# An early tile of the fullest expert between dense part and routed loop, and logits of three row tiles in three column groups

## The reference

```python
def _attn_ref(q, k, v, g_norm):
    kv = np.einsum('bhsd,bhse->bhde', k, v)
    out = np.einsum('bhsd,bhde->bhse', q, kv)
    rms = np.sqrt(np.mean(out * out, axis=-1, keepdims=True) + 1e-06)
    return out / rms * g_norm

def _moe_ref(x, domain_probs, w1, w2):            # every expert, every row
    p = domain_probs / (domain_probs.sum(-1, keepdims=True) + 1e-09)
    for e in range(E):
        out += p[:, e:e + 1] * (np.maximum(x @ w1[e], 0.0) @ w2[e])

def _moe2_ref(x, expert_emb, tau, w1, w2):        # one expert for each row
    logits = xn @ en.T / tau                      # xn, en: rows over their norms
    expert_idx = np.argmax(logits, axis=1)
    gate_w = softmax(logits)[np.arange(N), expert_idx]
    for e in range(E):
        mask = expert_idx == e
        out[mask] = gate_w[mask, None] * (np.maximum(x[mask] @ w1[e], 0.0) @ w2[e])
```

## Time and profile before

| | |
|---|---|
| runs before, median of 3 | 1151.87 us (1150.92 to 1154.58) |
| the profiled execution | 1151.53 us |
| its span | 1149.9 us, 18699 instructions |
| PE busy | 1125.5 us, 98% of the span |
| DVE, POOL, ACT busy | 728.5 (63%), 655.9 (57%), 455.3 us (40%) |
| mean granted clock of PE | 0.994 |
| HBM traffic | 218 GB/s over the span |

### The profile page before, as it was taken

One profiled execution on the slowest core, in us unless ns is written; L12 is line 12 of the kernel. 1 busy time (PEld: TensorE's weight loads), 2 busy tenths in 40 slices (PEclk: granted clock), 3 DMA queues, 4 the chain that ended last, 5 costly groups with the idle time before them and its releaser, 6 DMA issues.

```text
span 1149.9 us, 18699 instructions
## 1 busy us (share of the span) xinstructions
PE 1125.5 (98%) x6206; PEld 992.3 (86%) x6207; DVE 728.5 (63%) x1159; ACT 455.3 (40%) x808; POOL 655.9 (57%) x609
## 2 busy tenths in 40 slices
PE   8999999999999999999999999999999999999996
PEld 8888889999889888998889888998887788888885
DVE  4877888888976788888875878888662222222221
ACT  4773444444434444444434444444222222222220
POOL 1587777799867777899867777777330111111101
PEclk9999999999999999999999999999989999999998
DMA  9955777777512448877612448777369749427960
GB/s 245 268 157 180 267 268 271 278 275 276 199 45 78 142 131 302 289 278 261 216 37 75 137 146 302 279 273 270 144 243 383 273 183 372 153 100 302 374 238 13
DMA packets 102433, 250.87 MB, mean 218 GB/s; under 512 B 8254, under 2 KB 48190, under 8 KB 94171
## 3 DMA queue, kind: packets, MB, share of 16 engines
q1 hardware_dynamic: 97360, 235.18, 59.2%
q0 software_dynamic: 4800, 14.72, 3.7%
q10 hardware_dynamic: 203, 0.05, 0.0%
HBM read 170.99 MB, written 79.98 MB: 218 GB/s over the span
## 4 chain that ended last, share of the span: by engine, by line
PE 82%; DVE 7%; POOL 4%; issue 3%; DMA 2%; ACT 2%; SPq 0%; DVEq 0%; POOLq 0%; ACTq 0%
PE ps L1277 25%; PE ps L1279 25%; PE ps L1278 25%; PE ps L1466 2%; DMA w_raw<-in_moe_w_dram 1%; DVE x_rows L965 1%; POOL w_lo L483 1%; PE ps L1235 1%; PE ps L1432 1%; PE ps L1370 1%; DVE hT_lo L954 1%; PE ps L1205 1%; DVE attn_rows L887 1%; DVE x_ops_lo L978 1%; DVE hT_lo L952 0%
## 5 line engine op out<-in xcount | busy, mean ns | idle before, releaser
L1277 PE MATMUL ps<-x_ops_hi,w_hi 128*128 128x384 f32 x672 | 226.5, 337 | 3.4 <-DVE sum L935 3.2
L1277 PE MATMUL ps<-w_hi,hT_hi 128*128 128x512 f32 x576 | 227.1, 394 | 0.4
L1279 PE MATMUL ps<-x_ops_hi,w_lo 128*128 128x384 f32 x672 | 225.7, 336 | 0.0
L1279 PE MATMUL ps<-w_hi,hT_lo 128*128 128x512 f32 x576 | 225.4, 391 | 0.0
L1278 PE MATMUL ps<-x_ops_lo,w_hi 128*128 128x384 f32 x672 | 225.2, 335 | 0.0
L1278 PE MATMUL ps<-w_lo,hT_hi 128*128 128x512 f32 x576 | 225.0, 391 | 0.0
L965 DVE SCALAR_TENSOR_TENSOR x_rows<-ps,dense_probs,x_rows 128x512 f32<-128x512 f32 x270 | 189.8, 738 | 22.2 <-PE ps L1279 22.2
L608 POOL DMA_INDIRECT out_dram<-y_rows,row_ids x22 | 22.6, 1026 | 237.3 <-DVE y_rows L1168 141.9
L492 POOL TENSOR_TENSOR w_lo<-w_raw,w_hi 128x512 fp32r<-128x512 f32 x96 | 149.5, 1577 | 8.0 <-ACT w_hi L702 8.0
L1158 DVE TENSOR_TENSOR rhT_lo<-ps,rhT_hi 128x512 fp32r<-128x512 f32 x44 | 28.4, 686 | 172.9 <-ACT rhT_hi L826 172.9
L478 POOL TENSOR_TENSOR w_lo<-w_raw,w_hi 128x512 fp32r<-128x512 f32 x48 | 62.2, 1295 | 126.7 <-ACT w_hi L690 126.6
(11 more groups left out here) (198 smaller groups left out, 2006.8 us busy)
## 6 DMA issues: line engine op xcount, KB each, us to landing
w_slots<-split_parts SPq DMA_DIRECT2D x64, 1024.0 KB, 5.6
w_raw<-in_moe_w_dram SPq DMA_DIRECT2D x96, 512.0 KB, 3.5
ahead_raw<-in_moe_w_dram SPq DMA_DIRECT2D x64, 512.0 KB, 6.6
split_parts<-ahead_hi SPq DMA_DIRECT2D x64, 512.0 KB, 4.4
split_parts<-ahead_lo SPq DMA_DIRECT2D x64, 512.0 KB, 5.8
row_tile<-dispatched_rows POOLq DMA_DIRECT2D x20, 257.0 KB, 5.8
kv<-in_k_dram SPq DMA_DIRECT2D x16, 288.0 KB, 7.9
kv<-in_v_dram SPq DMA_DIRECT2D x16, 288.0 KB, 8.2
```

The source lines that it names most:

```text
L1277: mm(out_, ah, bh, start=(first and m == 0), stop=False, skip_group_check=not final or not first)
L1279: last = mm(out_, al, bh, start=False, stop=(final and m == n - 1), skip_group_check=not final or not first)
```

## The change

It does two things.

**An early tile.** At step 41, when twelve of the row tiles are routed and scattered, DVE picks the expert that leads (`choose_star`, 13 small instructions) and shifts that expert's region and tables by one tile. SP loads 128 of its rows; in the tail PE flips them, and ACT and DVE split them. SP loads the w1 of that expert (`load_early(0)`) into the pieces of the odd place ahead of the w1 of place 0, and after the last down product its w2 (`load_early(1)`). PE computes the tile where the fillers were, with pieces of the work between the last ranks; ReLU, copies and splits of it are placed between routing and table steps on ACT and DVE. `tile 0` is now this tile, the loop's tiles start with 1, and two of them are written out ahead of the loop. The w1 of place 1 and both w2 are loaded behind the first row tiles. The last six tiles' scatters count on a semaphore of their own.

**Logits of the first four blocks.** The embeddings, padded with zeros to 32 columns, are the stationary operand, and the flipped tiles move, 128 columns each. The three tiles of a block write to partitions 0, 32 and 64 of one bank. ACT copies the 96 x 128 result and PE transposes it once. The buffer of flipped tiles has three places in place of two. The last six tiles keep the old form.

The diff, cut to its core:

```diff
+            def load_early(m):
+                for c in range(PCS):
+                    n = (2 * m + 1) * PCS + c
+                    sp.dma_start(W[:, n * PIECE:(n + 1) * PIECE].bitcast(F32),
+                                 parts[e_star, :, (m * PCS + c) * PIECE:(m * PCS + c + 1) * PIECE]).then_inc(early_in[m][c // 2], 16)
...
                     fill_rows()
-            sp.wait_ge(up_done, OPS * STEPS)
+            sp.wait_ge(star_ready, 1)
+            e_star = sp.value_load(tab_s[0:1, 0:1], min_val=0, max_val=E2 - 1)
+            r_star = sp.value_load(tab_s[0:1, 1:2], min_val=P, max_val=E2 * CAP)
             for s in range(2):
                 sp.wait_ge(s_out[s], 32 * (NAHEAD // 2))
-            for n in range(2 * PCS):
-                load_first(n)
+            sp.wait_ge(scattered, 16 * T0)
+            sp.dma_start(xs[:, 0, :], rows[bass.ds(r_star, P), :]).then_inc(first_rows_in[0], 16)
+            sp.wait_ge(up_done, OPS * STEPS)
+            load_early(0)
+            load_first(0, 0)
...
@@ -402,17 +426,20 @@
             sp.wait_ge(h_lo, 4 * STEPS)
             sp.wait_ge(y_done, TPT * STEPS)
             sp.wait_ge(w2_split, STEPS)
+            load_early(1)
             sp.wait_ge(tab_ready, 1)
             first_rows = [sp.value_load(tab_r[0:1, s:s + 1], min_val=0, max_val=E2 * CAP + P) for s in range(2)]
-            sp.wait_ge(scattered, 16 * TT)
-            for s in range(2):
-                sp.dma_start(xs[:, s, :], rows[bass.ds(first_rows[s], P), :]).then_inc(first_rows_in[s], 16)
-            for s in range(2):
-                sp.wait_ge(first_rows_in[s], 16)
-            for n in range(2 * PCS, 4 * PCS):
-                load_first(n)
+            sp.wait_ge(scattered, 16 * T0)
+            sp.wait_ge(scattered_late, 16 * TPT)
+            sp.dma_start(xs[:, 1, :], rows[bass.ds(first_rows[0], P), :]).then_inc(first_rows_in[1], 16)
+            sp.dma_start(xs[:, 0, :], rows[bass.ds(first_rows[1], P), :]).then_inc(first_rows_in[2], 16)
+            sp.wait_ge(rh_done, 3)
+            load_first(1, 0)
+            load_first(0, 1)
+            sp.wait_ge(ry_done, 2)
+            load_first(1, 1)
...
+                        A(lgt[:, :], ps[0:3 * EW, 3, 0:P], ACT.Copy).then_inc(lgt_copied, 1)
                     if k == at_ + 1:
                         exponentials(b)
-            for t in range(TT - TPT, TT):
...
+            for s in range(2):
+                act.wait_ge(s_out[s], 32 * (NAHEAD // 2))
+            rx(0, 0)
+            for t in range(T0, TT):
                 route(t)
...
+            for half in range(2):
+                relu_half(0, half)
+                rt_half(0, 0, half)
             act.wait_ge(tab_ready, 2)
             tiles = act.value_load(tab_n[0:1, 0:1], min_val=TT, max_val=KT)
-            rx(0, 0)
             rx(1, 1)
-            relu_rows(0)
-            rt_parts(0, 0)
-            with act.Fori(0, PAIRS) as i:
+            rx(2, 0)
+            relu_rows(1)
+            rt_parts(1, 1)
+            rx(3, 1)
+            relu_rows(2)
...
+            V.memset(enT[:, :, :], 0.0).then_inc(enT_cleared, 1)
...
-                step(V.tensor_tensor(r_("logit", b), in_bank(2, b), wide(scl[:, slice(*BLOCKS[b])], b), ALU.mult))
+                found = ps[:, 2, HT:HT + 3 * EW].rearrange("p (t e) -> p t e", e=EW)[:, :, 0:E2] if b in ROUTE_AT else in_bank(2, b)
+                step(V.tensor_tensor(r_("logit", b), found, wide(scl[:, slice(*BLOCKS[b])], b), ALU.mult))
                 dve.sem_inc(lg_read, 1)
...
+            def choose_star():
+                dve.wait_ge(rank_read, NB - 3)
+                step(V.tensor_tensor(ecol[:, 0, :], run[:, :], ebase[:, :], ALU.subtract))
+                step(V.tensor_reduce(star_col[:, 0:1], ecol[:, 0, :], AX.X, ALU.max))
+                step(V.tensor_tensor(ecol[:, 1, :], ecol[:, 0, :], star_col[:, 0:1].to_broadcast([P, E2]), ALU.is_equal))
+                step(V.tensor_tensor(ecol[:, 1, :], ecol[:, 1, :], iota_e[:, :], ALU.mult))
+                step(V.tensor_reduce(star_col[:, 1:2], ecol[:, 1, :], AX.X, ALU.min))
+                step(V.tensor_tensor(star[:, :], iota_e[:, :], star_col[:, 1:2].to_broadcast([P, E2]), ALU.is_equal))
+                step(V.tensor_scalar(tab_s[:, 0:1], star_col[:, 1:2], float(E2), None, ALU.add))
+                V.tensor_scalar(tab_s[:, 1:2], star_col[:, 1:2], float(CAP), float(E2 * CAP + P), ALU.mult, ALU.add).then_inc(star_ready, 1)
+                step(V.tensor_scalar(jumps[:, :], star[:, :], float(-P), float(CAP), ALU.mult, ALU.add))
+                step(V.scalar_tensor_tensor(jumps[:, 0:E2 - 1], star[:, 1:E2], float(P), jumps[:, 0:E2 - 1], ALU.mult, ALU.add))
+                step(V.scalar_tensor_tensor(ebase[:, :], star[:, :], float(P), ebase[:, :], ALU.mult, ALU.add))
+                step(V.tensor_scalar(star_col[:, 2:3], star[:, 0:1], 1.0, float(P), ALU.add, ALU.mult))
+                step(V.tensor_scalar(kstart[:, :], knum[:, :], float(P), star_col[:, 2:3], ALU.mult, ALU.add))
...
             for k in range(STEPS):
                 t = k // NU
+                if k == STAR_AT:
+                    choose_star()
                 if k % NU == 0 and k:
                     for j in range(TPT):
...
             for n, (kk, j) in enumerate(TAIL):
                 add(kk, j)
+                if n == 2:
...
+            step(V.tensor_tensor(kc_(5), kstart[:, :], kc_(0), ALU.add))
...
             step(V.tensor_tensor(cmpo[:, :, :], ec(4).unsqueeze(1).to_broadcast(oe), knum[:, 0:E2].unsqueeze(2).to_broadcast(oe), ALU.is_le), False)
...
+            def first_results():
+                dve.wait_ge(gi_copied, 1)
+                V.tensor_copy(ids[:, 0:1], early_gi[:, 1:2])
+                dve.wait_ge(ry_done, 2)
+                V.tensor_scalar(ys[:, 0, :], ps[:, 5, :], early_gi[:, 0:1], None, ALU.mult).then_inc(ry_ready, 1)
...
+                if t == T0:
+                    pe.wait_ge(rx_split, 1)
                 if t >= 2:
...
+            def logits_by_tile(b, k):
+                pe.wait_ge(xt_copied, BLOCKS[b][1])
+                pe.wait_ge(c21_done, k + 1)
+                for c in range(KC):
+                    for g in range(3):
+                        last = mm(ps[g * EW:(g + 1) * EW, 3, 0:P], enT[:, c, :], xt[:, g, c * P:(c + 1) * P],
+                                  start=(c == 0), stop=(c == KC - 1))
+                last.then_inc(lgt_done, 1)
+            def logits_by_token(b, k):
+                pe.wait_ge(lgt_copied, b + 1)
+                pe.wait_ge(c12_done, k + 1)
+                if b:
+                    pe.wait_ge(lg_read, b)
+                tr(ps[:, 2, HT:HT + 3 * EW], lgt[:, :], ident[0:3 * EW, 0:3 * EW]).then_inc(lg_done, 3)
...
-                            if k == at_ and first <= first + j - 2 < end:
-                                logits(first + j - 2, k)
+                            if k == at_ and j == 4:
+                                logits_by_tile(b, k)
+                            if k == at_ and j == 5:
+                                logits_by_token(b, k)
                                 chosen = b + 1
...
+            def early_up(half, chunks):
+                pe.wait_ge(rx_split, 1)
+                pe.wait_ge(y_used, TPT * STEPS)
+                if half:
+                    pe.wait_ge(lg_read, NB)
+                for c in chunks:
+                    pe.wait_ge(early_in[0][c // (KC // 2)], 32)
+                    cs = slice(c * P, (c + 1) * P)
+                    m = 2 * WCOL + c // (KC // 2) * 2 * PIECE + c % (KC // 2) * F + half * 512
+                    last = three(ps[:, 1 + half, :], [(rxh[:, 0, cs], rxl[:, 0, cs], W[:, m:m + 512], W[:, PIECE + m:PIECE + m + 512])], c == 0, c == KC - 1)
+                if chunks[-1] == KC - 1:
+                    last.then_inc(rh_done, 1)
+            def flip_half(n, half):
+                pe.wait_ge(rh_relu, 2 * n + half + 1)
+                for c in range(4):
+                    m = half * 512 + c * P
+                    last = tr(ps[:, 3 + half, c * P:(c + 1) * P], hs[:, m:m + P], ident[:, :])
+                last.then_inc(rt_done, 1)
+            def early_down(chunks):
+                half = chunks[0] // (FCH // 2)
+                pe.wait_ge(rt_split, half + 1)
+                pe.wait_ge(early_in[1][half], 32)
+                for c in chunks:
+                    cs = slice(c * P, (c + 1) * P)
+                    m = 6 * WCOL + half * 2 * PIECE + c % (FCH // 2) * D
+                    last = three(ps[:, 5, :], [(rhh[:, 0, cs], rhl[:, 0, cs], W[:, m:m + D], W[:, PIECE + m:PIECE + m + D])], c == 0, c == FCH - 1)
+                if chunks[-1] == FCH - 1:
+                    last.then_inc(ry_done, 1)
             for n, (kk, j) in enumerate(TAIL):
                 down(kk, j)
+                if n == 1:
+                    pe.wait_ge(h_lo, 4 * LAST + 1)
+                    flip_rows(0, 0)
                 if n in (3, 5, 7, 9, 11):
```

(25 more changed lines are left out.)

189 lines of the change are left out of this document (105 added, 84 removed).

## The result

The change takes 1157.05 us (median of 9 runs, 1153.96 to 1161.83), the kernel before 1151.56 (9 runs): ratio 1.0049, 95% interval 1.0033 to 1.0065. It is slower by 5.5 us, where 1139.8 was forecast. The profiled execution has a span of 1155.3 us against 1149.9.

A forecast was written before the change was run, and what follows sets the result against it. PE, busy 98%, was taken as the bound, with a 14.5 us hole before the routed loop. -12.5 + 2.4 + 0.9 + 1.6 - 4.5 = -12.1 on 1151.53 gave 1139.4, as median 1139.8; range 1136.5 to 1147.0.

The forecast's parts named there:

- Logits, -4.5: First twelve tiles: three overlapping column groups replace the old logits products, saving 1.13 us a block, four times.
- serial: Rival, logits of the first twelve tiles: column groups run one after another, +2.3 in place of -4.5, 1146.6; chance 0.12.
- drain rival: Rival, logits blocks: switching the tiling mode empties PE's pipeline, 2.0 us in all, 1141.8; chance 0.10.
- Tail, +0.9: Last row tiles: four early transposes, a restart and a 0.3 us wait for DVE's split cost 0.9 us (0.5 to 1.5).
- Choosing the expert, +1.6: Step 41: 13 small DVE operations, 2.6 us, delay the first sum, so PE stands still 1.6 us (0 to 2.6).
- Hand-over, +2.4: Dense part to routed loop: early tile replaces fillers, scatter takes 6 us, first up product comes 2.4 us later (+0.7 to +5.3).
- The rival of the low clock: Hand-over: PE's wait of about 2 us for rows drops its clock, losing 3.4 us, 1143.2; chance 0.22.
- Loop start, 0: First loop tiles: 12 MB of weights follow the row DMAs from 861.3 and arrive just in time, cost 0.
- The rival had priced the right thing: Loop start: the weight stream binds; the gain is gone at 3.9 us a load, 1155.6 at 4.2; chance 0.04.
- One tile leaves the loop, -12.5: Routed loop: 21 tiles in place of 22, with steady tiles 12.52 us apart, saves 12.5 us.

The follow-up runs named there:

- logits_only: The kernel before with only the new logits of the first four blocks, no early tile: 1148.75 us, ratio 0.9972.
- star_alone: The kernel before plus the 13 expert-choosing instructions in one block ahead of step 41's adds, result unused: 1159.27 us, ratio 1.0064.
- star_rotated: Kernel before plus new logits, spread choosing, experts taken in turn from the fullest, whose first two loop tiles start early; no extra weight loads: 1140.77 us, ratio 0.9892.
- star_spread: The change with its 13 expert-choosing instructions spread in twos and threes between the adds of step 46: 1148.81 us, ratio 0.9982.
- place0_weights: The change with the choosing spread over step 46 and the early tile using place 0's weights, so 8 MB are not loaded: 1144.36 us, ratio 0.9932.

## Why the prediction was wrong

**Logits, -4.5 (bounds +2.3 to -5.3): mechanism right, size off.** Column groups run side by side: 24 products in 1.07 us, forecast 1.13, with no drain that would show (the serial and the drain rival both fell). `logits_only` gives -2.9. What the term lacked was who is late next: 2.0 us of PE's wait for POOL's norms, where 0.2 stood before.

**Tail, +0.9: about right.** From the fourth product of step 41 to the last logits the change takes 3.4 us more, `star_alone`, which has no early tile, 2.7 more (733.81 to 858.42); 0.7 is left.

**Choosing the expert, +1.6 (0 to 2.6): the first step that failed.** "Two such steps are 0.21 apart, 2.6 us" took a rate from a stretch where nothing stood against these instructions. The block took 5.8 us, PE waited 4.5 and then ran 6 us at the lower clock: 7.3 in `star_alone`. The upper bound was no bound. It is 5.7 of the 17.3 us of the miss, and I had no rival for it.

**Hand-over, +2.4 (0.7 to 5.3): the second.** It measured +7.3. The scatter was put at 6 us, with the upper bound at 9.0; it took 8.8. "The last one meets only the end of the stream" was wrong: the stream was to end about 858, and the early tile's second down half got its w2 at 867.32, which is 863.4 on the clock of before (the last logits stand 3.9 later). The early tile's down product waited 1.4 and 3.3 us for w2, which the term did not have at all, and the clock fell behind that. Windows of the change:

```profile
868.00:872.00 4.00, 2.98 (x12) 2.01 (x11) 0.00 (x0) 0.60 (x1) 0.00 (x0) 0.57 0.78 224
872.00:876.00 4.00, 4.00 (x14) 3.24 (x13) 2.15 (x5) 0.60 (x1) 0.68 (x2) 0.58 0.96 366
```

The rival of the low clock had the price about right, 3.4 us: 8 us at 0.575 are 3.4 at most, as PE stands still for 1.0 of them. Its trigger was another: it named the wait for the rows, and the products are slow from 868.57 on, behind the wait for w2 and ahead of that for the rows. It was not an alternative to the forecast, as I had it, but an addition to late waits.

**Loop start, 0, "with no room": the third.** Twelve loads from 868.48, which is 864.6 on the clock of before and not 861.3, make the products of the next tiles wait, 5.6 us in four waits, and the clock was 0.74 from 890 to 895, at most 1.3 us more. Together that is about the 6.6 us by which the loop gave less than the 12.5 of its tile. The rival had priced the right thing through the wrong cause: it asked for a load of 3.9 us, here the twelve issues took 36.97/11 = 3.4 us each, SP's own waits for the early products among them, and began 3.3 us late on that clock. A chance of 0.04 for a term with no room behind a chain of three uncertain delays was far too low.

**One tile leaves the loop, -12.5: right.** There are 21 stores behind the early one, in the steady part 12.5 us apart (1017.27, 1029.79). No run takes this term alone: `star_rotated` keeps its 22 tiles in the loop and gains by starting two of them early.

The sum failed in the hand-over also since its terms were added as if apart. They follow each other: w2 and the scatters delay one another, these delay the rows, the rows delay the weights behind them, and after some of the waits PE pays again in clock. The block at step 41 is no part of this chain as far as the runs show: taking it out gives back 8.2 by the medians (`star_spread`), and it costs 7.3 alone, 7.7 and 7.4 by the ratios. Of the 9.0 that are then left to the forecast, 4.5 are the additional 8 MB (`place0_weights`) and 1.6 the logits. That the remaining 2.9 are the late scatter was not isolated: the run meant for it moved the wait to w2.
